# GpSimd sums the raw values of three first pairs and ScalarE copies four pooled outputs, in a fused attention and two-layer expert kernel

## The chip, the core and the metric

The kernel runs on one core of a Trainium2 chip. A core has five instruction streams that run side by side and meet at semaphores: TensorE (PE in the profile, with its weight loads as PEld), VectorE (DVE), ScalarE (ACT), GpSimd (POOL) and SyncE (SP), which here only issues transfers. On-chip memory is SBUF; TensorE writes to PSUM, in eight banks. The metric is the device time of one launch in microseconds (us).

## What is computed

Attention over 4 batches, 8 heads, 576 positions and 64 values a head, once on keys and values pooled by four and once in a band of plus or minus 3 positions, then two feed-forward stages. Cut to what matters here:

```
q_d, k_d, v_d = mean over 4 neighbouring positions of q, k, v   # 576 -> 144 positions
out_d   = softmax(q_d @ k_d.T / 8) @ v_d
out_up  = repeat(out_d, 4)                                      # back to 576 positions
out_loc = softmax(q @ k.T / 8, only |i - j| < 4) @ v
x = out_up + out_loc                                            # 2304 tokens x 512
h = x @ w_in;   y = elu(h) @ w_out                              # 512 -> 2048 -> 512
z = (silu(y @ w_gate) * (y @ w_val)) @ w_out2                   # 512 -> 1536 -> 512
```

Everything is float32. The large products are done in three passes, on a high and a low part of each operand: ScalarE copies the high part, VectorE (or GpSimd) subtracts to get the low part.

## The kernel before

**Units.** Attention is cut into 48 units. A unit is one pair of heads (128 rows) on one group of 192 tokens; units 0 to 3 are the four pairs of the first group and form the prologue, which nothing else can cover, because the first feed-forward product needs their results. For a unit `u` the work goes round the engines:

- TensorE computes scores (`pe_scores`, L500 local, L512 pooled); VectorE adds the mask and finds maxima (`dve_masked_max`, L754 to L760); ScalarE takes exponentials (`act_exps`, L1056, L1060); VectorE normalises (`dve_normalise`, L765 to L772).
- TensorE transposes the probabilities (`pe_transposes`, L521); ScalarE copies them to SBUF (`act_copies`, L1068).
- TensorE multiplies with the values (`pe_outputs`): 6 local products on a window of V (L536, 12 instructions in the profile), and then the pooled output, in one of two ways. For pairs in `SUMMED_BY_PRODUCT` it multiplies with the raw values, 24 products (L546, 48 instructions), so that the sum over four positions is made by the product itself. For the others it multiplies with `v_pool`, values already pooled, 6 products (L558, 12 instructions), and waits for GpSimd's `v_pooled`.
- The pooled output is copied to `o_pool` (L777, VectorE), the local and the pooled parts are added to give `x_raw` (L781, VectorE), ScalarE copies the high part to `x_hl` (L1074) and VectorE makes the low part (L787). `o_pool` is a single buffer.

**GpSimd** pools the raw values `v_raw` of the first batch in the order `ORDER_V` (`pool_pool_v`, L1290: half sums in place, two instructions for each of three row blocks; L1294: three sums to `v_pool`). For a pair that TensorE multiplies raw, it first waits until TensorE has done so, since the half sums overwrite the raw values. The pooled values are used again by later groups of the same batch.

**The order.** There is no scheduler. Each engine's program is written out by hand: the prologue line by line, and then one loop over 112 steps (`STEPS`), each with a hidden product, an accumulation and slots for the units that follow. An engine runs its own list strictly in order, so an instruction that waits holds back all behind it. On TensorE the prologue ends with `pe_outputs` of units 1, 2 and 3, and then `pe_hidden` for steps 0 and 1: chunk `c` of it (three matmuls, L572 to L574) needs the high and low x of unit `c`, and step `s` needs its weight piece, made by ScalarE (`act_weight_a`, L1104) and VectorE (`dve_weight_low`, L793). The elu of a step is L1091 and L1093 (ScalarE) and L818 (VectorE), the parts of its result L1099 and L827.

**Transfers** are issued by SyncE in the order of its own list: keys, queries, raw values (`load_vraw`, L1373, four transfers a pair, 288 KB), windows (`load_vwin`, L1368), and weight pieces (`load_piece_a`, L1381, 256 KB). Weight pieces from number 20 on land where the prologue's buffers lie, so they wait for GpSimd's last pooled pair.

The calls on the three engines, in the prologue before:

```python
# VectorE
dve_normalise(dve, 2); dve_output(dve, 0); dve_normalise(dve, 3); dve_x_low(dve, 0)
dve_output(dve, 1); dve_weight_low(dve, 0); dve_x_low(dve, 1); dve_weight_low(dve, 1)
dve_output(dve, 2); dve_x_low(dve, 2); dve_weight_low(dve, 2); dve_output(dve, 3)
# TensorE
pe_outputs(pe, 0); pe_transposes(pe, 1); pe_transposes(pe, 2); pe_outputs(pe, 1)
pe_transposes(pe, 3); pe_outputs(pe, 2); pe_outputs(pe, 3); pe_hidden(pe, 0, range(0, 2))
```

## Time and profile before

| | |
|---|---|
| device time, median of 3 runs | 973.29 us (971.01 to 974.42) |
| the profiled execution | 971.3 us, its span 969.5 us |
| TensorE matmul busy | 959.9 us, 99% of the span |
| VectorE busy | 604.1 us, 62% |
| ScalarE busy | 385.6 us, 40% |
| GpSimd busy | 163.4 us, 17% |
| chain that ended last | TensorE 94%, ScalarE 3%, VectorE 2%, transfers 1% |

A row of the timeline has the start in us, the time from the first start to the last end of the merged instructions, the engine, the line, the operation, the tiles and, in brackets, how long the engine had sat idle and what ended that. Matmuls overlap one another, and the ends of matmuls are modelled. GpSimd's durations are rough: its starts are the better reading.

### The profile page before, as it was taken

The numbers are of one execution on the slowest core, as the hardware profiler recorded it, in microseconds if no ns is written. First come the engines' busy times: TensorE is split into PE (matmuls) and PEld (weight loads), VectorE is DVE, ScalarE is ACT, GpSimd is POOL, SyncE is SP. The second block draws the span as 40 slices with busy tenths as digits, with TensorE's granted clock in tenths as the row PEclk, the third lists the DMA queues.
The fourth block names the chain that finished last, engine by engine and source line by source line (L and its number), as shares of the span: only waits on it lengthen the run. The fifth ranks groups of instructions, "written<-read, shape, count | busy, mean of one in ns | idle before, by whom it ended". The sixth has DMA issues, their size and how long they took to land.

```text
span 969.5 us, 20170 instructions
## 1 busy us (share of the span) xinstructions
PE 959.9 (99%) x7916; PEld 908.1 (94%) x7917; DVE 604.1 (62%) x1364; ACT 385.6 (40%) x1027; POOL 163.4 (17%) x210
## 2 busy tenths in 40 slices
PE   8999999999999999999999999999999999999998
PEld 5889999999999999999999999999999999999998
DVE  7887656566555565555358884534759846667552
ACT  5776554344344443444335632232324422222221
POOL 7304510014000000000006920000008910000000
PEclk9999999999999999999999999999999999999999
DMA  9645531125110211110132301112023132120202
GB/s 250 186 127 109 99 58 47 27 73 106 27 39 26 75 51 31 60 37 8 56 108 87 99 23 44 45 44 67 1 87 123 58 103 88 44 87 23 88 11 77
DMA packets 55661, 67.88 MB, mean 70 GB/s; under 512 B 6760, under 2 KB 37832, under 8 KB 55568
## 3 DMA queue, kind: packets, MB, share of 16 engines
q1 hardware_dynamic: 48272, 62.76, 21.0%
q0 software_dynamic: 6816, 3.55, 2.7%
q8 instruction: 63, 1.03, 0.5%
q10 hardware_dynamic: 480, 0.30, 0.1%
q14 instruction: 30, 0.25, 0.1%
HBM read 52.42 MB, written 14.16 MB: 69 GB/s over the span
## 4 chain that ended last, share of the span: by engine, by line
PE 94%; ACT 3%; DVE 2%; DMA 1%; issue 1%; ACTq 0%; DVEq 0%
PE bank L572 29%; PE bank L573 28%; PE bank L574 28%; PE bank L536 2%; PE bank L500 2%; PE bank L521 2%; PE bank L558 1%; PE bank L512 1%; ACT weights L1104 1%; DMA q_sb<-qT 1%; DVE weights L793 1%; ACT prob L1060 1%; PE bank L546 0%; PE bank L487 0%; DVE g_sb L818 0%
## 5 line engine op out<-in xcount | busy, mean ns | idle before, releaser
L574 PE MATMUL bank<-x_hl,gv_hl 128*128 128x256 f32 x768 | 217.3, 283 | 0.0
L573 PE MATMUL bank<-x_hl,gv_hl 128*128 128x256 f32 x768 | 217.3, 283 | 0.0
L572 PE MATMUL bank<-x_hl,gv_hl 128*128 128x256 f32 x768 | 217.2, 283 | 0.0
L572 PE MATMUL bank<-x_hl,weights 128*128 128x384 f32 (+1 forms) x448 | 147.2, 329 | 2.0 <-DVE weights L793 1.8
L572 PEld LDWEIGHTS bank<-x_hl,gv_hl 128*128 128x128 f32 x768 | 147.3, 192 | 0.9
L573 PEld LDWEIGHTS bank<-x_hl,gv_hl 128*128 128x128 f32 x768 | 147.3, 192 | 0.9
L572 PE MATMUL bank<-g_hl,weights 128*128 128x384 f32 (+1 forms) x448 | 147.8, 330 | 0.3 <-DVE g_hl L827 0.2
L1315 POOL TENSOR_TENSOR gv_hl<-gv_raw,gv_hl 128x256 fp32r<-128x256 f32 x84 | 72.5, 898 | 447.9 <-ACT gv_hl L1110 447.9
L574 PEld LDWEIGHTS bank<-x_hl,gv_hl 128*128 128x128 f32 x768 | 147.3, 192 | 0.0
L573 PE MATMUL bank<-x_hl,weights 128*128 128x384 f32 (+1 forms) x448 | 143.4, 320 | 0.0
L574 PE MATMUL bank<-g_hl,weights 128*128 128x384 f32 (+1 forms) x448 | 143.3, 320 | 0.0
L574 PE MATMUL bank<-x_hl,weights 128*128 128x384 f32 (+1 forms) x448 | 143.2, 320 | 0.0
L573 PE MATMUL bank<-g_hl,weights 128*128 128x384 f32 (+1 forms) x448 | 143.2, 320 | 0.0
L820 DVE TENSOR_SCALAR g_sb<-g_sb 128x384 f32<-128x384 f32 x80 | 30.4, 380 | 106.8 <-ACT g_sb L1095 106.8
L572 PEld LDWEIGHTS bank<-g_hl,weights 128*128 128x128 f32 x448 | 84.5, 189 | 9.2 <-issue 8.7
L572 PE MATMUL bank<-u_hl,w_hl 128*128 128x512 f32 (+1 forms) x240 | 88.6, 369 | 0.0
L573 PE MATMUL bank<-u_hl,w_hl 128*128 128x512 f32 (+1 forms) x240 | 88.6, 369 | 0.0
L574 PE MATMUL bank<-u_hl,w_hl 128*128 128x512 f32 (+1 forms) x240 | 88.3, 368 | 0.0
L572 PEld LDWEIGHTS bank<-x_hl,weights 128*128 128x128 f32 x448 | 84.7, 189 | 3.4 <-DVE weights L793 3.0
L573 PEld LDWEIGHTS bank<-x_hl,weights 128*128 128x128 f32 x448 | 84.8, 189 | 0.0
L574 PEld LDWEIGHTS bank<-x_hl,weights 128*128 128x128 f32 x448 | 84.7, 189 | 0.0
L574 PEld LDWEIGHTS bank<-g_hl,weights 128*128 128x128 f32 x448 | 84.7, 189 | 0.0
(127 smaller groups left out, 1604.8 us busy)
## 6 DMA issues: line engine op xcount, KB each, us to landing
landing<-w SPq DMA_DIRECT2D x32, 256.0 KB, 4.8
x_raw<-yT_scratch SPq DMA_DIRECT2D x14, 512.0 KB, 4.5
v_win<-v_windows SPq DMA_DIRECT2D x46, 105.0 KB
q_sb<-qT SPq DMA_DIRECT2D x88, 48.0 KB, 2.3
partT_scratch<-out_sb SPq DMA_DIRECT2D x16, 256.0 KB, 2.2
out_sb<-partT_scratch SPq DMA_DIRECT2D x4, 1024.0 KB, 5.1
outT<-out_sb SPq DMA_DIRECT2D x16, 256.0 KB, 2.0
k_sb<-kT SPq DMA_DIRECT2D x14, 288.0 KB, 3.4
```

What stands on the lines that cost most here:

```text
L500: nc.tensor.matmul(x[rows, t * WIN:(t + 1) * WIN], q[:, half, t * QT:(t + 1) * QT], k[:, k0:k0 + WIN], start=True, stop=True)
L512: mm = nc.tensor.matmul(x[rows, LOC:SCORES], q_pool[:, u % 2, half, :], k_pool[:, p, :], start=True, stop=True)
L521: mm = nc.tensor.transpose(x[0:CHUNK, t * P:(t + 1) * P], prob(u)[:, t * CHUNK:(t + 1) * CHUNK], ident[:, :])
L536: nc.tensor.matmul(y[cols, t * QT:(t + 1) * QT], v[:, t, cols], pT[:, t * P + half * QT:t * P + (half + 1) * QT], start=True, stop=True)
L558: mm = nc.tensor.matmul(y[cols, GROUP:GROUP + PQ], v_pool[:, a % 2, p, c, cols], pT[:, at:at + PQ], start=(c == 0), stop=(c == TILES - 1))
L572: nc.tensor.matmul(out, w_hi, x_hi, start=first, stop=False)
L573: nc.tensor.matmul(out, w_hi, x_lo, start=False, stop=False)
L574: return nc.tensor.matmul(out, w_lo, x_hi, start=False, stop=last)
L793: nc.vector.tensor_tensor(piece(n, 1), raw(n), piece(n, 0).bitcast(F32), ALU.subtract).then_inc(w_lo_done, 1)
L820: nc.vector.tensor_scalar(g, g, 1.0, -1.0, ALU.min, ALU.add).then_inc(t_done, 1)
L1060: op = nc.scalar.activation(e, e, ACT.Exp, bias=neg_max[:, r, t:t + 1], scale=SCALE, accum_out=row_sum[:, r, t:t + 1])
L1315: nc.gpsimd.tensor_tensor(gv_hl[2 * p + j][:, 1, w, :], gv_raw[2 * p + j][:, w, :], gv_hl[2 * p + j][:, 0, w, :].bitcast(F32), ALU.subtrac ...
```

## The change

The pairs whose raw values TensorE multiplies are now pair 0 alone; GpSimd pools pairs 1, 2, 3 and then 0. GpSimd's half sums are one instruction of 256 values for each row block, not two of 128. The copy of the pooled output to `o_pool` moves for units 0 to 3 from VectorE to ScalarE. SyncE issues the raw values of pairs 2 and 3 earlier, and pieces that alias the prologue wait in addition for the outputs of its four units.

```diff
-ORDER_V = [1, 0, 2, 3]
-SUMMED_BY_PRODUCT = (0, 2, 3)
+ORDER_V = [1, 2, 3, 0]
+SUMMED_BY_PRODUCT = (0,)
...
         def dve_output(dve, u):
             y = bank_y(u)
-            dve.wait_ge(outputs_done, u + 1)
-            nc.vector.tensor_copy(o_pool[:, :], y[:, GROUP:GROUP + PQ]).then_inc(opool_copied, 1)
+            if u >= PROLOGUE:
+                dve.wait_ge(outputs_done, u + 1)
+                nc.vector.tensor_copy(o_pool[:, :], y[:, GROUP:GROUP + PQ]).then_inc(opool_copied, 1)
             wait(dve, x_hi_done, u - 1)
             wait(dve, x_lo_done, u - 1)
             dve.wait_ge(opool_copied, u + 1)
...
+        def act_first_pooled_output(act, u):
+            act.wait_ge(outputs_done, u + 1)
+            wait(act, x_done, u)
+            nc.scalar.activation(o_pool[:, :], bank_y(u)[:, GROUP:GROUP + PQ], ACT.Copy).then_inc(opool_copied, 1)
...
             act_copies(act, 1)
             act_copies(act, 2)
+            act_first_pooled_output(act, 0)
             act_x_high(act, 0)
             act_copies(act, 3)
+            act_first_pooled_output(act, 1)
             act_x_high(act, 1)
             act_weight_a(act, 1)
             act_weight_a(act, 2)
+            act_first_pooled_output(act, 2)
             act_x_high(act, 2)
             act_weight_a(act, 3)
+            act_first_pooled_output(act, 3)
             act_x_high(act, 3)
...
             for c in range(TILES):
-                for h in range(2):
-                    cols = slice(DH * h, DH * h + DH)
-                    nc.gpsimd.tensor_tensor(x[:, c, 0:2, cols], x[:, c, 0:2, cols], x[:, c, 2:4, cols], ALU.add).then_inc(v_half_sums, 1)
+                nc.gpsimd.tensor_tensor(x[:, c, 0:2, :], x[:, c, 0:2, :], x[:, c, 2:4, :], ALU.add).then_inc(v_half_sums, 1)
             pool.wait_ge(zero_rows_set, 3)
-            pool.wait_ge(v_half_sums, 2 * TILES * (i + 1))
+            pool.wait_ge(v_half_sums, TILES * (i + 1))
...
                 sp.wait_ge(v_pooled, PAIRS)
+                sp.wait_ge(outputs_done, PROLOGUE)
...
             load_vraw(sp, 0)
+            load_vraw(sp, 2)
             load_vwin(sp, 1)
+            load_vraw(sp, 3)
             load_vwin(sp, 2)
-            load_vraw(sp, 2)
             load_piece_a(sp, 0)
             load_vwin(sp, 3)
-            load_vraw(sp, 3)
```

What it does to the order on TensorE, at the end of the prologue (bank5 holds the outputs of unit 2, bank1 those of unit 3; the row before these is the transposes of unit 3):

```order
 L536 MATMUL bank5<-probT_first_110,v_win_first_107 64x64 x6
-L546 MATMUL bank5<-probT_first_110,v_raw_108 64x48 x24
+L558 MATMUL bank5<-probT_first_110,v_pool_85 64x48 x6
 L536 MATMUL bank1<-probT_first_110,v_win_first_107 64x64 x6
-L546 MATMUL bank1<-probT_first_110,v_raw_108 64x48 x24
+L558 MATMUL bank1<-probT_first_110,v_pool_85 64x48 x6
 L572 MATMUL bank4<-x_hl_99,weights_49 128x192
```

Two groups of 24 products become two of 6, which read what GpSimd has written; nothing else moves on TensorE.

ScalarE, from the copies of the transposed probabilities of units 1 and 2 on, before:

```order
L1068 ACTIVATE probT_first_110<-bank2 118x384
L1068 ACTIVATE probT_first_110<-bank4 118x384
L1074 ACTIVATE x_hl_99<-x_raw_98 128x192
L1068 ACTIVATE probT_first_110<-bank0 118x384
L1074 ACTIVATE x_hl_99<-x_raw_98 128x192
L1104 ACTIVATE weights_49<-landing2_52 128x512
L1104 ACTIVATE weights_49<-landing4_54 128x512
L1074 ACTIVATE x_hl_99<-x_raw_98 128x192
```

and after:

```order
L1069 ACTIVATE probT_first_110<-bank2 118x384
L1069 ACTIVATE probT_first_110<-bank4 118x384
L1074 ACTIVATE o_pool_92<-bank7 128x48
L1080 ACTIVATE x_hl_99<-x_raw_98 128x192
L1069 ACTIVATE probT_first_110<-bank0 118x384
L1074 ACTIVATE o_pool_92<-bank3 128x48
L1080 ACTIVATE x_hl_99<-x_raw_98 128x192
L1110 ACTIVATE weights_49<-landing2_52 128x512
L1110 ACTIVATE weights_49<-landing4_54 128x512
L1074 ACTIVATE o_pool_92<-bank5 128x48
L1080 ACTIVATE x_hl_99<-x_raw_98 128x192
```

The copy for unit 0 stands behind the copies for units 1 and 2, that for unit 1 behind the copy for unit 3, and that for unit 2 behind two weight pieces. (L1074 is the new copy in the kernel after; L1068, L1074 and L1104 of before are L1069, L1080 and L1110 there.)

VectorE at the same place, from the addition for unit 0 on, before and after:

```order
L777 COPY o_pool_92<-bank7 128x48
L781 TENSOR_TENSOR x_raw_98<-bank7,o_pool_92 128x192
L765 TENSOR_SCALAR row_inv_96<-row_sum_95 128x4
L767 RECIPROCAL row_inv_96<-row_inv_96 128x4
L770 TENSOR_TENSOR prob_first_109<-prob_first_109,row_inv_96 128x3x70
L772 TENSOR_SCALAR prob_first_109<-prob_first_109,row_inv_96 128x3x48
```

```order
L782 TENSOR_TENSOR x_raw_98<-bank7,o_pool_92 128x192
L765 TENSOR_SCALAR row_inv_96<-row_sum_95 128x4
L767 RECIPROCAL row_inv_96<-row_inv_96 128x4
L770 TENSOR_TENSOR prob_first_109<-prob_first_109,row_inv_96 128x3x70
L772 TENSOR_SCALAR prob_first_109<-prob_first_109,row_inv_96 128x3x48
```

The addition for unit 0 now waits for ScalarE's copy, and the normalising of unit 3 (the last four rows) still stands behind it.

## Rows read from the trace of the kernel before

**Rows 1.** Stages: busy us and instructions of each engine, clock, transfer share, GB/s.
```profile
5.60:9.30 3.70, 1.56 (x28) 1.11 (x28) 1.74 (x4) 1.61 (x7) 0.69 (x1) 1.00 1.07 242
18.80:25.40 6.60, 6.25 (x154) 5.54 (x153) 5.90 (x16) 3.79 (x9) 6.38 (x13) 1.00 1.02 330
34.40:90.00 55.60, 53.13 (x609) 49.81 (x607) 43.16 (x130) 40.94 (x141) 8.62 (x12) 1.00 0.44 121
90.00:969.00 879.00, 876.83 (x6924) 836.44 (x6920) 534.46 (x1160) 326.29 (x825) 128.24 (x146) 1.00 0.21 60
```

**Rows 2.** Timeline of TensorE, end of the prologue and start of the hidden products.
```profile
17.12 1.60 PE L546 MATMUL bank<-probT_first,v_raw 48*64 48x48 f32 x48
...
20.23 0.54 PE L558 MATMUL bank<-probT_first,v_pool 118*64 118x48 f32 x12
20.70 0.54 PE L521 MATMUL bank<-ident,prob_first 128*118 128x128 f32 x3
...
21.67 1.76 PE L546 MATMUL bank<-probT_first,v_raw 48*64 48x48 f32 x48
...
23.86 1.60 PE L546 MATMUL bank<-probT_first,v_raw 48*64 48x48 f32 x48
25.39 0.36 PE L572 MATMUL bank<-x_hl,weights 128*128 128x192 f32 x1
...
27.49 0.33 PE L572 MATMUL bank<-x_hl,weights 128*128 128x192 f32 x1
```

**Rows 3.** Timeline of VectorE: end of unit 2's normalising, copies and additions.
```profile
18.08 0.31 DVE L772 TENSOR_SCALAR prob_first<-prob_first,row_inv 128x144 f32<-128x144 f32 x1
18.77 0.21 DVE L777 COPY o_pool<-bank 128x48 f32<-128x48 f32 x1 [0.37 <-PE bank L546]
19.01 0.36 DVE L781 TENSOR_TENSOR x_raw<-bank,o_pool 128x192 f32<-128x192 f32 x1
...
19.98 0.51 DVE L772 TENSOR_SCALAR prob_first<-prob_first,row_inv 128x144 f32<-128x144 f32 x1
...
21.16 0.36 DVE L781 TENSOR_TENSOR x_raw<-bank,o_pool 128x192 f32<-128x192 f32 x1
...
26.20 0.36 DVE L781 TENSOR_TENSOR x_raw<-bank,o_pool 128x192 f32<-128x192 f32 x1
26.99 0.36 DVE L787 TENSOR_TENSOR x_hl<-x_raw,x_hl 128x192 fp32r<-128x192 f32 x1 [0.43 <-ACT x_hl L1074]
```

**Rows 4.** Timeline of ScalarE: a small copy, and the copies around the new ones.
```profile
7.00 0.24 ACT L1187 ACTIVATE mask<-band 64x70 f32<-64x70 f32 x1
...
19.23 0.87 ACT L1068 ACTIVATE probT_first<-bank 118x384 f32<-118x384 f32 x2 [0.87 <-PE bank L521]
...
21.28 0.49 ACT L1068 ACTIVATE probT_first<-bank 118x384 f32<-118x384 f32 x1 [0.93 <-PE bank L521]
```

**Rows 5.** Timeline of GpSimd: half sums and sums of the first pair, then the second.
```profile
12.86 2.73 POOL L1290 TENSOR_TENSOR v_raw<-v_raw 48x128 f32<-48x128 f32 x6
15.73 1.28 POOL L1294 TENSOR_TENSOR v_pool<-v_raw 48x128 f32<-48x128 f32 x3
18.88 2.86 POOL L1290 TENSOR_TENSOR v_raw<-v_raw 48x128 f32<-48x128 f32 x6 [1.87 <-PE bank L546]
...
33.05 1.28 POOL L1294 TENSOR_TENSOR v_pool<-v_raw 48x128 f32<-48x128 f32 x3 [0.50 <-POOL v_raw L1290]
```

**Rows 6.** One line's instructions: duration in ns, min/median/max, first and last start.
```profile
L1290 POOL TENSOR_TENSOR v_raw<-v_raw x24: 446/452/960, 12.9 to 32.1; 48x128 f32<-48x128 f32 x24
L1315 POOL TENSOR_TENSOR gv_hl<-gv_raw,gv_hl x84: 727/912/1195, 513.5 to 773.6; 128x256 fp32r<-128x256 f32 x84
L772 DVE TENSOR_SCALAR prob_first<-prob_first,row_inv x4: 309/412/512, 14.8 to 20.0; 128x144 f32<-128x144 f32 x4
L793 DVE TENSOR_TENSOR weights<-landing,weights x32: 677/685/959, 21.4 to 80.9; 128x512 fp32r<-128x512 f32 x32
```

**Rows 7.** The first weight piece's transfer, issued at 10.71 us, from issue to landing.
```profile
DMA to landing us min/median/max: 6.2/6.2/6.2
```

## The prediction

> **What bounds the kernel now.** I first cut the run into stages. From 90 us to the end TensorE is busy 876.83 of 879.00 us [rows 1]: nothing there waits, and nothing there is edited. So the change can only move the start of that stage, and each microsecond gained or lost ahead of it is gained or lost at the end. Between 34.4 and 90 us TensorE is busy 53.13 of 55.60 us [rows 1], so at most 2.5 us of idle time there could soak up a delay; ScalarE and VectorE take turns there and pace TensorE in most of its gaps, and they start from the same hidden products, so I expect them to pass a delay on, not to absorb it. What is edited lies between 12.9 and 34.3 us. The second view is the timeline of that stretch, engine by engine. TensorE has hardly a gap in it (6.25 of 6.60 us busy from 18.8 to 25.4 [rows 1]): it goes from the raw products of unit 2 (21.67) to those of unit 3 (23.86) and straight into the hidden products at 25.39; chunk 3 of step 0, the first that needs x of unit 3, starts at 27.49 [rows 2], right behind VectorE's low part of that x, which starts at 26.99 and takes 0.36 [rows 3]. So two things end there together: TensorE's own list, and VectorE's. That is the point of the case. The change shortens the first. What it does to the second decides.
>
> **The change, part by part.**
>
> *TensorE.* Two groups of 48 small matmuls, 1.76 and 1.60 us, become two of 12, 0.54 us each [rows 2]. That takes 3.36 - 1.08 = 2.3 us off TensorE's list. It is a gain only if nothing else is late at 27.49.
>
> *The copy on ScalarE.* VectorE copies unit 0's pooled output at 18.77, as soon as the raw products end (17.12 + 1.60 = 18.72), and adds at 19.01 [rows 2, 3]. ScalarE's copy costs as much: no ScalarE copy of 48 columns is in the trace, and the nearest row, 70 columns, took 0.24 [rows 4]. But it stands behind the copies for units 1 and 2, which wait for the transposes and run from 19.23 to 20.10 [rows 4]. So it ends at about 20.3, and the addition starts there and not at 19.01: 1.3 us later. Queued behind that addition on VectorE is the normalising of unit 3, which ended at 19.98 + 0.51 = 20.49 [rows 3]; it now ends at 20.49 + 1.3 = 21.8. For its transposes TensorE waits: 20.70 [rows 2] becomes 21.8, 1.1 us later. ScalarE's copy of these goes from 21.28 [rows 4] to 22.4, and its new copy for unit 1 stands behind: 22.4 + 0.4 (half of the 0.87 of two such) + 0.24 = 23.05. The addition for unit 1 was at 21.16 [rows 3]: 1.9 us later.
>
> From there VectorE's list is additions, low parts of x and low parts of weights, nearly back to back to the addition for unit 3, 26.20 - 21.16 = 5.04 us [rows 3]. The change takes from it the copies for units 2 and 3. From copy to addition were 0.24 us for unit 0 [rows 3]; with the slot at the front I take 0.3 each, 0.6 in all. ScalarE's copies for units 2 and 3 run while VectorE is on weights, and cost nothing there. So the last addition and the last low part of x come 1.9 - 0.6 = **1.3 us later**, and chunk 3 of step 0 starts at 28.8 instead of 27.49. TensorE's 2.3 us then lie idle: it is ready early and waits.
>
> *GpSimd, when pair 3 is ready.* A half sum of 256 values isn't in the trace for this tile. Instructions of 128 start 0.41 us apart (five distances in 2.73 less the last one's 0.45, which holds one longer distance), so at 0.83 a wide one would gain nothing; the nearest row of 256 values, with GpSimd undisturbed, is 727 ns, against 446 for 128 [rows 6]. I take 0.69 from start to start (0.41 + the difference, 0.28). A pair is then 3 x 0.69 + 0.14 + 1.28 = 3.5 us undisturbed [rows 5], and 5.15 us if it is disturbed as the last three pairs were ((34.33 - 18.88) / 3 [rows 5]). The wait of 1.87 us [rows 5] for unit 0 is gone, as pair 0 now comes last. Three pairs from 12.86 are done between 23.4 and 27.3 (the first one was hardly disturbed, 17.01 - 12.86 = 4.15 us), and I take 24.5, as the wider instructions save 0.4 a pair and VectorE waits in between. The products of unit 3 then end at 25.0, and chunks 0 to 2 of two steps, 27.49 - 25.39 = 2.1 us of work [rows 2], are done at 27.1, ahead of 28.8. So GpSimd is covered by VectorE's lateness up to 26.2 us; past that it costs one for one.
>
> *Beside each other.* GpSimd stood idle from 17.0 to 18.88 [rows 5], exactly while VectorE normalised units 1 and 2. Now it works through this. Beside GpSimd the last step of normalising took 512 ns, undisturbed 309 [rows 6], and a weight's low part 959 instead of 677 [rows 6]. With two to four such collisions of 0.2 to 0.3 us on units 1 and 2, the normalising of unit 2 moves from 18.39 [rows 3] to between 18.8 and 19.6, against transposes that TensorE reaches at about 18.72 + 0.4 = 19.1: 0 to 0.5 us. GpSimd's instructions are also twice as wide, so each collision from 18.9 to 27 us can cost up to 0.28 us more; some four of them lie on VectorE's path, up to 1.1. I take **0.8 us**, from 0 to 1.8. The other way, GpSimd is done at about 28.5 instead of 33.05 + 1.28 = 34.3 [rows 5], and two weight instructions and two low parts between 29 and 34 run undisturbed: up to 4 x 0.28 = 1.1 us on VectorE, of which I take **-0.5**, as the elu chain there also waits for ScalarE and TensorE.
>
> The rule that bears on this is in the Trainium skill, SBUF — State Buffer, section Who interferes with whom: an instruction of VectorE with two inputs in SBUF and one of GpSimd that reads SBUF share a read port as an exclusive lock, and the second to issue blocks until the first is through. By that rule, a wider instruction holds VectorE back for its whole length; the 512 against 309 ns agree with it for narrow ones.
>
> *SyncE.* Raw values of pair 3 now go ahead of weight piece 0, one more pair of 288 KB. At the 330 GB/s of that stretch [rows 1] (less while small packets run) this is 0.9 to 1.3 us. Piece 0 landed at 10.71 + 6.2 = 16.9 [rows 7] and now lands at about 18.1; ScalarE takes it between the exponentials of unit 3 and 19.23, where it has 0.9 us free, so it costs nothing up to 18.6, and beyond that delays the copies for units 1 and 2 one for one. The added wait on the outputs is met long before the first aliased piece is due: nothing.
>
> **Sum.** 1.3 + 0.8 - 0.5 = +1.6 us. The profiled execution took 971.3 us (span 969.5), so it becomes 972.9; the median of the runs is 973.29, 2.0 us more, and becomes 974.9.
>
> **The rivals.**
>
> *TensorE's saving comes through (faster).* If ScalarE's copy of unit 0 slipped in with the others (at 19.6 and not 20.0), or TensorE's wait at transposes were shorter than I think, VectorE's list would be only 0.3 to 0.5 us late, the 0.6 us for two copies would pay it back, and the end of outputs would decide: unit 3's products end at 24.5 instead of 25.46. Together with 0.5 from the earlier end of GpSimd that is -0.9 to -1.5 us, say 972.1. For it speaks that TensorE really was continuous; against it the order of ScalarE's list, which the diff fixes. It decides from the point where the addition for unit 1 starts before 21.9.
>
> *The port (slower).* If each wide instruction blocks VectorE for its whole length, then eight of its instructions up to 27 us (two in the normalisings, six after) each wait some 0.4 us: 3.2 us in place of 0.8, and the total is +4.0, 977.3. It decides from three such full waits on. Against it: the median of GpSimd's half sums, 452 ns, is hardly above their shortest, 446 [rows 6], so most met nothing. The rule of the Trainium skill cited above is this rival.
>
> *The clock (slower).* TensorE would be idle for up to 2 us of the stretch from 21 to 28. If its granted clock fell from 2.4 to 1.2 GHz, the hidden products of steps 0 and 1, 24 matmuls at 2.1 / 18 = 0.117 us each [rows 2], 2.8 us, would take 5.6, so +1.6 + 2.8 = +4.4, 977.7. Against it: from 5.6 to 9.3 us TensorE was busy only 1.56 of 3.70 us, and the granted clock stayed at 1.00 [rows 1].
>
> *GpSimd bounds.* With pair 3 ready at 27.3, the upper end above, the products of unit 3 end at 27.8 and chunk 3 starts at 29.9: +2.4 - 0.5 = +1.9, 975.2.
>
> **Chances.** The forecast 0.56, GpSimd as the bound 0.13, TensorE's saving 0.14, the port 0.11, the clock 0.06. A measurement of this kernel can tell about 0.3% from no change, 2.9 us. The forecast, GpSimd and the saving lie within it; the port and the clock don't, and I add a little for the runs' own spread (971.01 to 974.42): faster by over 0.3% 0.03, within 0.80, slower 0.17. The range has the saving at its lower end and the port at its upper, 971.7 to 978.0, which also takes in the ends of the unknown terms (+0.2 to +3.1).
>
> **What would show it.** Right: in the timeline of after, ScalarE's copy of unit 0 stands at about 20.1 behind two copies, VectorE's addition for unit 0 at 20.3 and for unit 1 near 23; TensorE has idle time ahead of the transposes of unit 3 and ahead of chunk 2 or 3, put down to VectorE or ScalarE and not to GpSimd; chunk 3 starts at 28.5 to 29.5; from 34 us on all rows stand later by one amount. Wrong: TensorE goes into the hidden products before 25 and into chunk 3 before 27.4 (the saving came through), or idles on GpSimd ahead of unit 3's products past 26.2, or the clock is below 1.00 in the stretch.

## The result: 2.2 us slower, within the forecast's bound of no change

The changed kernel took 974.63 us, the median of 22 runs (971.87 to 976.28); the kernel before, run beside it, took 971.55 us (22 runs, 969.82 to 974.42). The ratio is 1.0023, with a 95% interval of 1.0014 to 1.0031: 2.2 us slower, 1.4 to 3.0, and below the 0.3% (2.9 us) that the forecast set as its bound, which the upper end of the interval just passes. The forecast time of 974.9 us is met to 0.3 us, and part of that is luck: the three runs it started from had a median of 973.29, some 1.7 us above that of the 22 runs, and the step it forecast was +1.6 us where the medians are 3.1 apart.

Every run lists its mean granted clock: the clock that TensorE was given, as a share of full speed (2.4 GHz), over the whole run. Here the two kernels differ. All 22 runs of after are below 1.000. The kernel before was run 93 times beside the experiments, and 50 of those were at 1.000.

| granted clock | before: runs, mean us | after: runs, mean us |
|---|---|---|
| 1.000 | 50, 971.00 | none |
| 0.998 | 15, 972.79 | 6, 972.86 |
| 0.996 | 22, 973.32 | 6, 974.72 |
| lower | 6 (0.997 once), 976.08 | 10, 975.10 |

The profiled execution of after took 976.28 us, at the upper end of its runs. The windows of TensorE, as in [rows 1] (busy us, instructions, granted clock, transfer share, GB/s):

```profile
5.60:9.30 3.70, 1.89 (x27) 0.98 1.03 252
9.30:12.90 3.60, 3.59 (x30) 0.54 0.92 169
...
18.80:25.40 6.60, 4.97 (x122) 1.00 1.05 329
25.40:30.00 4.60, 2.31 (x26) 0.96 0.74 227
30.00:34.40 4.40, 4.40 (x32) 0.50 0.00 2
...
90.00:969.00 879.00, 879.00 (x6953) 1.00 0.21 60
```

Three things answer to [rows 1]. From 18.8 to 25.4 us TensorE is busy 4.97 us where it was 6.25: the saved products turned into idle time. From 30.0 to 34.4 its granted clock is 0.50, the 1.2 GHz level. And from 90 us on it is as full as before, so nothing is given back later. GpSimd's later line shows by how much everything moved (duration min/median/max in ns, first and last start); it was 513.5 in [rows 6]:

```profile
L1323 POOL TENSOR_TENSOR gv_hl<-gv_raw,gv_hl x84: 727/914/1195, 518.4 to 778.6; 128x256 fp32r<-128x256 f32 x84
```

Now the timelines, against [rows 2]. TensorE:

```profile
18.67 1.60 PE L546 MATMUL bank<-probT_first,v_raw 48*64 48x48 f32 x48
...
23.72 0.52 PE L521 MATMUL bank<-ident,prob_first 128*118 128x128 f32 x3 [1.40 <-DVE prob_first L772]
...
25.28 0.54 PE L558 MATMUL bank<-probT_first,v_pool 118*64 118x48 f32 x12
26.38 0.36 PE L572 MATMUL bank<-x_hl,weights 128*128 128x192 f32 x1 [0.57 <-DVE weights L794]
...
29.24 0.33 PE L572 MATMUL bank<-x_hl,weights 128*128 128x192 f32 x1 [1.41 <-DVE x_hl L788]
...
30.88 0.41 PE L572 MATMUL bank<-x_hl,weights 128*128 128x192 f32 x1
31.09 0.41 PE L573 MATMUL bank<-x_hl,weights 128*128 128x192 f32 x1
...
31.52 0.41 PE L572 MATMUL bank<-x_hl,weights 128*128 128x192 f32 x1
```

All its waits of over 0.3 us are for VectorE, none for GpSimd. From 30.88 on the matmuls start 0.21 us apart; at the upper clock such matmuls start 0.11 apart. Chunk 3 of step 0 starts at 31.52 instead of 27.49. ScalarE, against [rows 4], and VectorE, against [rows 3]:

```profile
20.79 0.93 ACT L1069 ACTIVATE probT_first<-bank 118x384 f32<-118x384 f32 x2 [0.87 <-PE bank L521]
21.61 0.21 ACT L1074 ACTIVATE o_pool<-bank 128x48 f32<-128x48 f32 x1
```

```profile
21.85 0.36 DVE L782 TENSOR_TENSOR x_raw<-bank,o_pool 128x192 f32<-128x192 f32 x1 [1.32 <-ACT o_pool L1074]
...
23.03 0.55 DVE L772 TENSOR_SCALAR prob_first<-prob_first,row_inv 128x144 f32<-128x144 f32 x1
...
25.17 1.15 DVE L794 TENSOR_TENSOR weights<-landing,weights 128x512 fp32r<-128x512 f32 x1
26.25 0.89 DVE L788 TENSOR_TENSOR x_hl<-x_raw,x_hl 128x192 fp32r<-128x192 f32 x1
...
30.39 0.36 DVE L788 TENSOR_TENSOR x_hl<-x_raw,x_hl 128x192 fp32r<-128x192 f32 x1 [0.43 <-ACT x_hl L1080]
```

The chain of the forecast is there: two transposes' copies, then the new copy, then the addition, then unit 3's normalising. Not in it is the 1.55 us by which all of this starts later. The raw products of unit 0 begin at 18.67 instead of 17.12. A transfer of queries made TensorE start 0.2 us later at 9.0, and the rest was lost while it ran at 0.54 from 9.3 to 12.9 us, ahead of every instruction that the change touches on TensorE. This start-up differs from execution to execution: in the profiles of the eleven experiments the raw products begin between 16.1 and 16.9 (six), between 17.0 and 17.7 (four), and at 18.68, there with the clock at 1.00 up to that point. So from here on I count from the start of unit 0's products. The low part of x of unit 3 then comes 30.39 - 18.67 = 11.72 us behind it, before 26.99 - 17.12 = 9.87. I call this distance the **list length**; after is 1.85 above before. It can itself differ between executions with the same lists ahead of it: two of the experiments below gave 10.67 and 11.26 (copies earlier, without and with fillers), and the difference was there before the first filler. After and the run with ten fillers agree to 0.1.

### The profile page after: what moved, and what is told of

It is laid out like the page before. It is cut to its first block, busy times and chain, and to the rows that moved or that the text cites. A ratio compares the mean times of both kernels' runs of the same rounds, so it can differ in the third digit from the quotient of the medians.

```text
span 974.5 us, 20027 instructions
## 1 busy us (share of the span) xinstructions
PE 962.6 (99%) x7844; PEld 909.5 (93%) x7845; DVE 602.8 (62%) x1360; ACT 385.8 (40%) x1031; POOL 159.5 (16%) x198
## 4 chain that ended last, share of the span: by engine, by line
PE 93%; ACT 3%; DVE 2%; DMA 1%; issue 1%; ACTq 0%; DVEq 0%
PE bank L572 29%; PE bank L573 28%; PE bank L574 28%; PE bank L536 2%; PE bank L500 2%; PE bank L521 2%; PE bank L558 1%; PE bank L512 1%; ACT weights L1110 1%; DMA q_sb<-qT 1%; PE bank L487 1%; DVE weights L794 1%; ACT prob L1061 1%; DVE g_sb L819 0%; ACT g_sb L1099 0%
## 5 line engine op out<-in xcount | busy, mean ns | idle before, releaser
L572 PEld LDWEIGHTS bank<-x_hl,weights 128*128 128x128 f32 x448 | 85.8, 192 | 5.7 <-DVE weights L794 3.3
L573 PEld LDWEIGHTS bank<-x_hl,weights 128*128 128x128 f32 x448 | 86.0, 192 | 0.0
L574 PEld LDWEIGHTS bank<-x_hl,weights 128*128 128x128 f32 x448 | 85.8, 192 | 0.0
```

What stands on the lines that cost most here:

```text
L572: nc.tensor.matmul(out, w_hi, x_hi, start=first, stop=False)
L573: nc.tensor.matmul(out, w_hi, x_lo, start=False, stop=False)
L574: return nc.tensor.matmul(out, w_lo, x_hi, start=False, stop=last)
```

## The experiments

I had two theories. **Order**: the place of ScalarE's copies, and VectorE waiting behind them, make the whole delay. **Clock**: in TensorE's new gaps the granted clock falls, and that makes a share of it. A third candidate is GpSimd's wide instructions beside VectorE's. Ratios below are to the kernel before, run beside them, with 95% intervals.

**The copy alone, and the pooling alone.** The first makes the change's edits to `dve_output` and to ScalarE's list, and keeps GpSimd, SyncE and the order of pairs as before:

```
 ORDER_V = [1, 0, 2, 3]
 SUMMED_BY_PRODUCT = (0, 2, 3)
```

> Only the copy of the pooled outputs of units 0 to 3 is moved to ScalarE; GpSimd, TensorE and SyncE do what they did before. Order theory (the copy stands behind others on ScalarE, and the normalising of unit 3 behind the addition on VectorE): the addition of unit 0 comes 1.0 to 1.3 us later relative to the end of unit 0's products, so do the transposes of unit 3 and, as TensorE still has its raw products behind them, the first hidden product; +1.2 to +1.4 us in all, clock at 1.00 from 20 us on, since TensorE has one gap of 1.1 us only. Port theory (VectorE is late because GpSimd works beside it and in wider instructions): 0 to +0.3 us. Clock theory (the cost is mostly the lower clock): 0 to +0.5 us.

Measured: 973.84 us (971.32 to 977.4), ratio 1.0017 [1.0001, 1.0033]. Its profile had the clock at 1.00 and its unit 0 products at 17.14, as before, so its VectorE rows can be laid beside [rows 3] without any shift:

```profile
20.26 0.36 DVE L782 TENSOR_TENSOR x_raw<-bank,o_pool 128x192 f32<-128x192 f32 x1 [1.85 <-ACT o_pool L1074]
...
23.06 0.36 DVE L782 TENSOR_TENSOR x_raw<-bank,o_pool 128x192 f32<-128x192 f32 x1 [1.06 <-ACT o_pool L1074]
...
28.05 0.36 DVE L788 TENSOR_TENSOR x_hl<-x_raw,x_hl 128x192 fp32r<-128x192 f32 x1 [0.43 <-ACT x_hl L1080]
```

The working said 20.3, 23.05 and 28.3. The list length is 10.91, +1.04; everything later stands 1.0 us later to the end. This is order, a little under its forecast size (+1.04 where +1.2 to +1.4 was expected), with half sums and clock as before. In the timed runs the clock was at 1.000 in 5 of 12 only, where it had been expected to hold; these five have a mean of 972.06, 1.04 above the 971.02 of before's runs at 1.000 in the same series.

The other half, GpSimd's sums with the copies left on VectorE:

```
         def dve_output(dve, u):
+            dve.wait_ge(outputs_done, u + 1)
+            nc.vector.tensor_copy(o_pool[:, :], y[:, GROUP:GROUP + PQ]).then_inc(opool_copied, 1)
-            act_first_pooled_output(act, 0)
...
-            act_first_pooled_output(act, 3)
```

> Only the pooling is changed (order of pairs, wide half sums, 6 products for units 2 and 3, SyncE's order); VectorE still copies. Order theory: the transposes of unit 3 are 0.7 to 1.0 us late, by collisions with GpSimd during the normalising of units 1 to 3, VectorE's weights and low parts then decide, chunk 3 of step 0 is 1 to 1.6 us late; +1.0 us with the clock held, up to +2.5 where TensorE's idle time of some 2 us makes the clock fall. Port theory: as late as the kernel after, +2.5 to +3.1 us, since the copy had no part in it. A theory that the products saved come through: -0.5 to -1 us.

Measured: 972.92 us (971.35 to 975.71), ratio 1.0014 [1.0001, 1.0027]. List length 10.83, +0.96, and the addition for unit 1 at 21.93, 0.8 later: with no copy moved, VectorE is held up by GpSimd alone. The three runs at clock 1.000 have a mean of 971.83, 0.8 above before's at 1.000. In its profile the clock fell, one stretch earlier than in after (TensorE's windows):

```profile
18.80:25.40 6.60, 4.85 (x87) 1.00 0.86 252
25.40:30.00 4.60, 3.62 (x20) 0.71 1.00 315
30.00:37.60 7.60, 7.60 (x46) 0.50 0.55 170
```

So each half lengthens the list by about 1 us, and the two together give 1.85, nearly their sum.

**Matmuls of constants in TensorE's gaps.** The changed kernel, with TensorE kept at work where it waited. `pe_filler` is in the kernel before too, where it fills gaps ahead of unit 0's outputs (L487). In this run and the two others with added fillers, SyncE's weight pieces from number 20 on wait in addition for the first hidden product, as they land where the constants lie:

```
+            pe_filler(pe, 5)
             pe_transposes(pe, 3)
...
             pe_hidden(pe, 0, range(0, 2))
+            for _ in range(5):
+                nc.tensor.matmul(bank_x(PROLOGUE - 1)[:, :], filler[:, 0:P], filler[:, :], start=True, stop=True)
             pe_hidden(pe, 0, range(2, 3))
...
                 sp.wait_ge(outputs_done, PROLOGUE)
+                sp.wait_ge(hid_done, 1)
```

> The kernel after, with 5 filler matmuls of 512 columns ahead of the transposes of unit 3 and 5 more ahead of chunk 2 of step 0, 1.1 us each time, where TensorE was idle for 1.40 and 1.41 us. Clock theory: the granted clock stays at 1.00 from 20 to 40 us, the hidden products of steps 0 and 1 and the scores of unit 4 run at 0.11 us and not 0.21 us a matmul, and the run is 1.5 to 2.2 us shorter than the kernel after, +0.9 to +1.6 us against before. If the fall of the clock had another cause (chance, the load of the other engines), it falls here too and the time is that of the kernel after, +3.1, or some tenths more.

Measured: 973.61 us (972.69 to 974.29), ratio 1.0018 [1.0006, 1.003]. All 12 runs had a granted clock of 1.000, where the changed kernel had none in 22, and their spread fell from 4.4 to 1.6 us. Windows of TensorE, the same stretches as above:

```profile
18.80:25.40 6.60, 5.10 (x86) 1.00 0.84 274
25.40:30.00 4.60, 4.12 (x35) 1.00 0.84 269
30.00:34.40 4.40, 4.20 (x46) 1.00 0.39 95
```

The list is as long as in after (11.80), so the fillers did nothing to the order up to there; what differs is the clock. From 41 to 780 us its profile stands 0.81 us later than before, of which its earlier start takes 0.55: net 1.36. In after the same sum is 4.97 - 1.55 = 3.4. The difference, **2.1 us, is the price of the lower clock in TensorE's gaps** in that one execution, the longest of its 22.

Its own total, 973.12, also holds 1.0 us from a load of weights that landed late at 780 us. ScalarE waited 10.60 us for it, in the profile with twelve fillers (below) 10.11, and in the other eleven profiles 9.07 to 9.39. The waits from 745 to 800 us (total, times, longest), here and in the kernel before:

```profile
ACT w_hl L1123 <- DMA w_raw<-w: 10.6, 1, 10.6
...
ACT w_hl L1114 <- DMA w_raw<-w: 9.2, 1, 9.2
```

Whether the fillers bring this about, or the wait that came with them, no run tells.

The timed runs give the clock a smaller part than the profile does. The expectation had the run 1.5 to 2.2 us shorter than the changed kernel; the median is 1.0 shorter, the mean 0.8 (973.59 against 974.38). And the kernel before loses time by the clock as well: the mean of its 22 runs beside the changed kernel is 972.01, and its runs at 1.000 have 971.00. So with the clock held in both the difference is 973.59 - 971.00 = 2.6 us, and without it 974.38 - 972.01 = 2.4: by this pair of runs the clock adds nothing to the difference. An estimate free of fillers comes from the two halves (the copy alone, the pooling alone) in their five and three runs at clock 1.000, 1.04 + 0.81 = 1.85 us above before; then the clock costs the changed kernel 974.38 - 972.85 = 1.5 us and before 1.0, and its share of the 2.4 is about 0.5. The changed kernel has no run at 1.000 that could settle it.

**ScalarE's copies earlier.** The copy for unit 0 ahead of the two transposes' copies, and the one for unit 1 ahead of those of unit 3:

```
+            act_first_pooled_output(act, 0)
             act_copies(act, 1)
             act_copies(act, 2)
-            act_first_pooled_output(act, 0)
             act_x_high(act, 0)
+            act_first_pooled_output(act, 1)
             act_copies(act, 3)
-            act_first_pooled_output(act, 1)
```

> The kernel after, with ScalarE's copy for unit 0 ahead of the copies of the transposed probabilities of units 1 and 2, and that for unit 1 ahead of those of unit 3. Order theory: the addition of unit 0 follows the end of its products by 0.3 us and not 1.57, the transposes of unit 3 come 0.7 to 1.3 us earlier, the addition of unit 1 by 1.2 to 1.9 us, chunk 3 by 1.2 to 1.5, and with shorter gaps the clock falls less often: 1.2 to 2.5 us less than the kernel after, +0.6 to +1.9 against before. Port theory: less than 0.4 us gained, as GpSimd still collides with VectorE throughout.

Measured: 972.36 us (971.25 to 973.69), ratio 1.0003 [0.999, 1.0016]: it can't be told from the kernel before. VectorE adds for unit 0 at 19.12, 2.2 us behind the start of unit 0's products; it was 1.9 in before, and 3.1 with the copy alone. List length 10.67, +0.80. Clock 1.000 in 7 of 12 runs; their mean of 971.74 is 0.7 above that of before's runs at 1.000, so most of the loss is gone, not all. Its TensorE still waits, in shorter gaps:

```profile
21.27 0.52 PE L521 MATMUL bank<-ident,prob_first 128*118 128x128 f32 x3 [0.57 <-DVE prob_first L772]
...
23.73 0.56 PE L558 MATMUL bank<-probT_first,v_pool 118*64 118x48 f32 x12 [0.71 <-POOL v_pool L1302]
...
25.86 0.33 PE L572 MATMUL bank<-x_hl,weights 128*128 128x192 f32 x1 [0.73 <-DVE x_hl L788]
...
28.36 0.33 PE L572 MATMUL bank<-x_hl,weights 128*128 128x192 f32 x1 [0.94 <-DVE x_hl L788]
```

The second row shows the next thing in line: with VectorE less late, the products of unit 3 wait for GpSimd's third pair, which the changed kernel's own lateness covers, as the forecast had it.

**Normalising of unit 3 ahead of unit 0's addition**, the other cure for the same wait:

```
             dve_normalise(dve, 2)
+            dve_normalise(dve, 3)
             dve_output(dve, 0)
-            dve_normalise(dve, 3)
```

> The kernel after, with VectorE's normalising of unit 3 ahead of the addition for unit 0. Order theory, by its second step (what is queued behind the waiting addition is what reaches TensorE): TensorE's idle time ahead of the transposes of unit 3 goes from 1.40 us to 0.2 to 0.5, chunk 3 of step 0 starts 1.0 to 1.4 us earlier counted from the products of unit 0, the clock falls less or not at all; 1.2 to 2.5 us less than the kernel after. If the later items of VectorE's list (weights, additions) alone decide, the transposes come earlier but chunk 3 doesn't, and less than 0.5 us is gained.

Measured: 975.11 us (973.22 to 975.34, only 5 runs), ratio 1.0033 [1.002, 1.0046]. The list shrank to 10.62 (+0.75), so the step on order holds in the trace, but the time is no better than the changed kernel's: no run was at clock 1.000, four of five at 0.995 or 0.993. The expectation had been 1.2 to 2.5 us less than the changed kernel. As a test of time this one speaks against order as the only cause.

**No half sums.** GpSimd leaves out the half sums, so the pooled values are sums of half the rows; nothing else is left out:

```
-            for c in range(TILES):
-                nc.gpsimd.tensor_tensor(x[:, c, 0:2, :], x[:, c, 0:2, :], x[:, c, 2:4, :], ALU.add).then_inc(v_half_sums, 1)
```

> The kernel after without GpSimd's half sums of the raw values (left out, so the pooled values of the first batch are the sum of two rows in four). GpSimd is done with all pairs by about 20 us and doesn't meet VectorE from then on. It measures the share of the collisions: by the sum of the prediction they are 0.8 of 2.1 us ahead of chunk 3, less 0.5 for relief that is gone to the same place, so chunk 3 comes 0.6 to 1.2 us earlier than in the kernel after and still about 1 to 1.3 us later than before, counted from unit 0's products. Port theory (VectorE is late mainly through GpSimd): chunk 3 comes 2 us earlier and the time is that of before. Order theory alone: less than 0.4 us gained.

Measured: 971.96 us (970.51 to 978.2), ratio 0.9998 [0.9982, 1.0015]. List length 10.44 against 11.72: the half sums beside VectorE cost **1.28 us** in the changed kernel, a little over the 0.6 to 1.2 expected. Its VectorE rows have the same instructions as those of after at 25.17 and 26.25, undisturbed:

```profile
23.45 0.68 DVE L794 TENSOR_TENSOR weights<-landing,weights 128x512 fp32r<-128x512 f32 x1
24.05 0.35 DVE L788 TENSOR_TENSOR x_hl<-x_raw,x_hl 128x192 fp32r<-128x192 f32 x1
```

0.68 against 1.15 and 0.35 against 0.89. These 1.28 us aren't what the change costs, since the kernel before pays for its own half sums too. The change's share is what the pooling adds: 11.72 - 10.91 = 0.81 us over the copy alone, or 0.96 by the pooling alone.

**Narrow half sums.** The changed kernel with each sum of 256 values as two of 128:

```
+                for h in range(2):
+                    cols = slice(DH * h, DH * h + DH)
+                    nc.gpsimd.tensor_tensor(x[:, c, 0:2, cols], x[:, c, 0:2, cols], x[:, c, 2:4, cols], ALU.add).then_inc(v_half_sums, 1)
```

> The kernel after with GpSimd's half sums as two instructions of 128 values each, as before. If the width is what costs (each collision holds VectorE for up to 0.55 us and not 0.28), VectorE's stretched instructions (low parts of weights, normalising) shrink and chunk 3 comes 0.5 to 0.9 us earlier. Against that GpSimd needs 0.4 us more a pair and has pair 3 ready at 25 to 26 us: then TensorE waits for GpSimd ahead of the products of unit 3, and the two nearly cancel: within 0.8 us of the kernel after either way. GpSimd bounds: 0.5 to 1.5 us longer than the kernel after.

Measured: 974.25 us (972.81 to 980.76), ratio 1.0028 [1.0015, 1.0041]. List length 11.71, the same as wide, but not for the same reason. Up to the low part of unit 2 the narrow form is 0.89 us ahead: 25.01 - 16.14 = 8.87 us behind the start of unit 0's products, against 28.43 - 18.67 = 9.76 in after and 25.99 - 17.46 = 8.53 without half sums. It loses that again by GpSimd's own time. The third pair is ready 25.42 - 11.88 = 13.54 us after GpSimd's first half sum, against 10.94 wide, TensorE waits for it ahead of the pooled products of unit 3 (9.3 us behind the start of unit 0's, against 6.6 in after), and ScalarE's copy and VectorE's addition wait behind these:

```profile
25.01 0.63 DVE L788 TENSOR_TENSOR x_hl<-x_raw,x_hl 128x192 fp32r<-128x192 f32 x1 [0.43 <-ACT x_hl L1080]
...
25.48 0.80 PE L558 MATMUL bank<-probT_first,v_pool 118*64 118x48 f32 x12 [2.70 <-POOL v_pool L1304]
...
27.07 0.36 DVE L782 TENSOR_TENSOR x_raw<-bank,o_pool 128x192 f32<-128x192 f32 x1 [0.56 <-ACT o_pool L1074]
```

So the width does cost, about the 0.5 to 0.9 us of the expectation, and the two nearly cancel, as it said. This rests on one profile of each form.

**Lists reordered.** If order is the cause, lists built for the new durations should win more than is lost: normalising 3 first, both first additions together, weights behind them, on ScalarE copies 0 and 1 together. TensorE's list is that of the changed kernel:

```
             dve_normalise(dve, 3)
             dve_output(dve, 0)
             dve_output(dve, 1)
             dve_weight_low(dve, 0)
             dve_weight_low(dve, 1)
             dve_x_low(dve, 0)
...
             act_copies(act, 1)
             act_first_pooled_output(act, 0)
             act_first_pooled_output(act, 1)
             act_x_high(act, 0)
```

> A try at a kernel that beats both: the kernel after, with each engine's prologue in the order in which its inputs come. VectorE: normalising of unit 3, additions for units 0 and 1, low parts of weights 0 and 1, then low parts and additions of the others, weight 2 last. ScalarE: each new copy as soon as its outputs are there, weight pieces behind. TensorE's list as in the kernel after. Order theory: chunk 3 of step 0 starts about when it did before or up to 0.3 us earlier counted from unit 0's products, and the two weight instructions that TensorE doesn't need come after; -0.5 us against before if the clock holds (-0.9 to +0.3), 2 to 3.5 us less than the kernel after. If GpSimd's collisions decide, it is no better than the copies-first version, +0.5 to +1.

Measured: 972.62 us, ratio 1.0008 [0.999, 1.0027], but in two groups: five runs at clock 1.000 with a mean of 970.34, below the 971.12 of before's runs at 1.000 in the same series, and seven below 1.000, nearly all of 973.6 or more. Its profile caught one of these. Windows of TensorE:

```profile
17.00:24.90 7.90, 5.64 (x101) 0.98 1.04 315
24.90:38.60 13.70, 13.70 (x109) 0.52 0.52 147
```

13.7 us at the lower level, and 976.75 us. Its list length of 10.61 was taken with the clock at this level from 24.9 on, so it doesn't give the order's share. No other run shows the two theories apart so well: the same instructions in the same order, 970.3 at clock 1.000 and 974.7 on average below it.

**Lists reordered, with fillers**, to hold the clock. Four matmuls of constants ahead of the transposes of unit 2, two ahead of those of unit 3, three ahead of unit 2's outputs, three ahead of chunk 2 of step 0:

```
+            pe_filler(pe, 4)
             pe_transposes(pe, 2)
             pe_outputs(pe, 1)
+            pe_filler(pe, 2)
             pe_transposes(pe, 3)
+            pe_filler(pe, 3)
             pe_outputs(pe, 2)
```

> The lists of VectorE, ScalarE and TensorE as in the run with reordered lists, and TensorE gets twelve matmuls of constants where it waited there: four ahead of the transposes of unit 2, two ahead of those of unit 3, three ahead of unit 2's outputs, three ahead of chunk 2 of step 0 (0.22 us each at the high level). Clock theory: the run with reordered lists came out in two groups, 969.97 to 971.65 and 973.59 to 977.03, and its profile, of the later group, showed the clock at its lower level from 24.9 to 38.6 us; if the clock is what tells the groups apart, the later group goes away: granted clock 1.00 (0.98 at least) from 20 to 40 us in the profile, all runs between 969.5 and 972, median near 970.7, which is 0.8 to 1.7 us under the kernel before. Rival, the order of the lists: the reordered lists gain nothing of their own and the early group was chance; the median stays between 972 and 974 with the clock held.

Measured: 971.61 us (970.61 to 972.18), ratio 0.9994 [0.9981, 1.0007]. The clock was 1.000 in 12 of 12 runs and the upper group is gone. The list length is 8.93, 0.94 below before:

```profile
18.80:25.40 6.60, 6.55 (x97) 1.00 0.93 288
25.40:30.00 4.60, 4.41 (x48) 1.00 0.87 275
```

The clock theory is right about the clock, and the time is 0.9 above what it gave: the mean of 971.55 is 1.2 above the 970.34 of the same lists at clock 1.000 without fillers (five runs, in another series). Its profile, of the shortest run, doesn't show fillers in the way. At 772 us it stands 1.2 us ahead of before (772.01 against 773.19 for the same instruction of VectorE, L908 in before), and of that 0.5 is lost where the load of weights lands late at 780, as in the run with ten fillers. What makes up the rest in the other runs is open. It is faster than the changed kernel. From the kernel before it can't be told.

**The kernel before with the normalising of unit 3 first** (the exchange of the changed kernel's run above, in the old kernel):

```
+            dve_normalise(dve, 3)
             dve_output(dve, 0)
-            dve_normalise(dve, 3)
```

> The kernel before with one exchange in VectorE's list: the normalising of unit 3 stands ahead of unit 0's copy and addition. The two raw sums of 48 small matmuls stay. Order theory: in the kernel before, the normalising stands 0.5 us behind its scores being ready, so its transposes come 0.5 to 0.7 us earlier, but TensorE is busy with the raw products of unit 2 until then, and the low parts of x follow the additions at the same time as before: 0 +- 0.5 us, 971.5 to 972.5, and chunk 3 of step 0 at 27.2 to 28.0. Clock theory: the raw products keep TensorE busy, so the clock stays at 1.00 from 20 to 40 us. Rival: the exchange by itself is a gain, which then has nothing to do with the change: under 970.8.

Measured: 970.74 us (970.36 to 973.59), ratio 0.9991 [0.9976, 1.0005]. List length 9.71, -0.16, so little to gain in the list, as order had it. The median is 0.8 under the expected range and at the rival's bound, but before's own runs beside it have a median of 971.35, also under that range, and the interval takes in no change. Eight of 12 runs at clock 1.000, as often as before's 18 of 29 beside it.

**Copies earlier, with fillers** (the run with the copies earlier, that is those of units 0 and 1, and five matmuls of constants, two ahead of the transposes of unit 3 and three ahead of chunk 2 of step 0):

```
+            pe_filler(pe, 2)
             pe_transposes(pe, 3)
```

> The changed kernel with ScalarE's copies for units 0 and 2 each placed ahead of the copies or exponentials they queued behind, as in the run with the copies first, and five matmuls of constants in TensorE's gaps (two ahead of the transposes of unit 3, three ahead of chunk 2 of step 0). Order and clock together: with the lists' delay taken back (that run had 0.6 us left) and the clock held at 1.00 from 20 to 40 us, the time is that of the kernel before within 0.5 us, 971.5 to 972.5, with no run above 974. Rival, the clock costs nothing in the other runs: the median is the same as with the copies first alone, 972.4, and the spread too (971.25 to 973.69).

Measured: 971.99 us (971.0 to 975.13), ratio 1.0006 [0.9989, 1.0022]. The median is where it was expected, but two runs were above 974 (974.15 at clock 1.000, and 975.13), and three of 12 runs were at 0.996, with a mean of 973.95, so five small matmuls made it likelier that the clock holds (9 of 12, against 7) and not certain; with 12 runs each, that difference alone is no proof.

## Why the prediction was right, and where it was not

*Where TensorE's saving goes.* Right. 2.3 us came off its list, all of it became waiting for VectorE (1.40 ahead of the transposes of unit 3), and the rival by which it comes through is out.

*ScalarE's copy and what queues behind it.* Right, to 0.1 us up to the addition for unit 1, in the run that holds all else still (the copy alone): addition for unit 0 at 20.26 (20.3 forecast), transposes of unit 3 at 21.89 (21.8), addition for unit 1 at 23.06 (23.05). The low part of unit 3 came +1.06 (+1.3). The 0.6 taken back by two copies fewer was 0.8: from the addition for unit 1 to the low part of unit 3 it is 4.99 us, before 26.99 - 21.16 = 5.83.

*GpSimd's wide sums.* Right. Three instructions took 2.08 us, so 0.69 from start to start. The third pair was ready at 24.39 (24.5), which is partly luck: GpSimd began 0.6 us later than in before (13.45) and took 10.94 us where the forecast had 11.6:

```profile
20.79 2.08 POOL L1298 TENSOR_TENSOR v_raw<-v_raw 48x256 f32<-48x256 f32 x3
23.01 1.38 POOL L1302 TENSOR_TENSOR v_pool<-v_raw 48x128 f32<-48x128 f32 x3
```

*Beside each other.* Right: 0.8 forecast, and the list of after is 0.81 longer than that of the copy alone. Leaving the sums out gives back 1.28, but part of that before paid too (959 ns in [rows 6], 0.51 in [rows 3]), and only the difference counts. Both of its reasons hold: GpSimd works through a stretch in which it used to stand idle, and wide sums cost more than narrow ones (9.76 against 8.87 us up to the low part of unit 2). The port rival had the mechanism right, one instruction at a time: a weight's low part went from 0.68 to 1.15, a low part of x from 0.35 to 0.89. Eight of VectorE's instructions between 18 and 27.2 us of after were held back, by 0.19 to 0.54 each, so by 0.3 on average and not by 0.4; what the rival left out is what before paid. The Trainium skill (SBUF — State Buffer, Who interferes with whom) has the second of the two blocked until the first is through; a wide sum takes 0.72, and the delays of up to 0.54 agree with that. The forecast's own example, 512 against 309 ns, is an instruction with one input tensor and one value a row (L772), not the two-tensor kind that its sentence on the rule names; the low parts above are of that kind.

*The relief afterwards.* -0.5 forecast; in the run with ten fillers the list was +1.93 and the rows from 41 us on +1.36: -0.57. Right.

*SyncE.* Right at nothing in after: no engine waits for weight piece 0, and ScalarE takes it at 19.29 without idle time, 1.55 us later than in before by the late start. In two experiments with an earlier start ScalarE did wait for it, 0.61 us (narrow sums) and 0.36 (copies earlier, with fillers).

*The sum of the order.* +1.6 forecast, +1.4 in the profile with ten fillers. The rows of after stand 4.97 us later than those of before: 1.55 by the start-up, 1.36 if its lists cost what they did in that run, and what is left over, 2.06, I put down to the clock.

*The clock.* This step failed. I gave it a chance of 0.06 on one row: before, TensorE was busy only 1.56 of 3.70 us from 5.6 to 9.3, and the clock stayed at 1.00 [rows 1]. That was one execution. In the profile of after the same untouched stretch reads 1.89 of 3.70, and the next 3.6 us were granted at 0.54. The copy alone has 1.89 of 3.70 there too, and its clock held. The same stretch did both, so one row in which the clock held was no evidence that it would. Nor did I see that before itself falls below 1.000 in 43 of 93 runs. In all 22 runs of after the clock fell somewhere; where is seen in the profiled one alone, and there it fell twice, once at the start and once in the hidden products, as the rival had it. The second fall cost 2.1 us (the rival had 2.8), I think because part of the slowed work was waiting for VectorE anyway, which no run tested. The forecast had also named a clock below 1.00 in the stretch as a sign of being wrong, and this sign came. As a bound from the timed runs: the mean granted clock was 0.9955 for after and 0.9984 for before, and 0.0029 of 971 us is 2.8 us of TensorE's work at most. By the estimate further up, the clock's share in the difference of the means is nearer to 0.5, because before pays for it too.

The verdict and the range hold: +2.2 is under the bound of 2.9 us, and the range had been drawn over the other cases. That the time of 974.9 is met so closely, with a clock term left at nothing and a starting median 1.7 us too high, is luck.

## What to carry to other kernels

Work taken from an engine that is not late becomes idle time, and idle time on TensorE is not always free: here all 22 runs had a stretch at the lower clock, and none of 12 with its gaps filled. What it costs must be read from many runs: in the one profile it was more than the lists did (2.1 against 1.4 us), over the timed runs less. A step moved to another engine costs its place in that engine's list, not its duration: 0.2 us of copy came 1.3 us late, and placing it two steps earlier took most of the loss back. And when one execution shows the clock holding through a gap, look at the granted clock of all runs before taking it for a rule.

## What the runs showed of the hardware

- The granted clock differs between executions of one program. One program with fixed lists (the reordered ones) ran at 1.000 in 5 of 12 runs and below in 7, 970.3 against 973.6 to 977.0 in nearly all. What TensorE did before the stretches at the lower level: busy 1.89 of 3.70, 2.11 of 4.40 (after), 5.64 of 7.90 with gaps of up to 0.99 us (reordered). Busy 1.56 of 3.70 (before), 1.89 of 3.70 (the copy alone) and 3.19 of 4.60 (copies earlier) were followed by none.
- With ten or twelve matmuls of constants in TensorE's gaps 24 of 24 runs were at 1.000; with five, 9 of 12; with none, 7 of 12 (copies earlier), 5 of 12 (reordered) and 0 of 22 (after).
- A GpSimd sum of 256 values takes 0.69 from start to start, two of 128 0.41 each. Up to the low part of unit 2 VectorE's list was 9.76 us beside wide sums, 8.87 beside narrow ones and 8.53 without any. GpSimd is held back too: its longest wide sum took 1179 ns, where most took 719:

```profile
L1298 POOL TENSOR_TENSOR v_raw<-v_raw x12: 714/719/1179, 13.4 to 25.7; 48x256 f32<-48x256 f32 x12
```
